# Tokens of the last chunk kept in their own order and stored by another queue; the first 1024 tokens gathered by index

## The reference

```python
# 1. attention: 16 neighbours on each side, and 24 blocks of 32 keys (max of k, mean of v)
x = attention(q, k, v)                       # 1536 tokens x 512
# 2. experts: each token goes to one of 8
expert_idx = np.argmax(logits, axis=1)
gate_w = probs[np.arange(N), expert_idx]
for e in range(E):
    mask = expert_idx == e
    h = np.maximum(x[mask] @ w1[e], 0.0)     # 512 -> 1024
    out[mask] = gate_w[mask, None] * (h @ w2[e])
# 3. one more network, the same for all tokens
h = x @ w_in                                 # 512 -> 2048
P = a[0] + a[1] * h + a[2] * h2 + a[3] * h3  # h2 = h*h, h3 = h2*h
Q = 1.0 + np.abs(b[0]) * np.abs(h) + np.abs(b[1]) * h2
return (P / (Q + 1e-06)) @ w_out             # 2048 -> 512
```

## Time and profile before

| | us |
|---|---|
| median of 3 runs | 735.77 |
| lowest and highest | 734.84 and 739.65 |
| the profiled execution | 735.92 |
| its span, from the first to the last instruction | 734.4 |
| mean granted clock of TensorE | 0.978 of 2.4 GHz |

### The profile page before, as it was taken

The page is one execution under the profiler, slowest core; times in us unless marked ns, Lnnn a source line. Parts: engine busy times, 40 slices in busy tenths (PEclk is TensorE's granted clock), DMA queues, the critical chain, the costliest instruction groups (busy, mean ns, idle before and its releaser), DMA issues.

```text
span 734.4 us, 11488 instructions
## 1 busy us (share of the span) xinstructions
PE 684.3 (93%) x3415; PEld 547.5 (75%) x3415; DVE 498.1 (68%) x976; ACT 417.7 (57%) x786; POOL 171.8 (23%) x232
## 2 busy tenths in 40 slices
PE   4779999999789999899999999999999999999991
PEld 4457777777567878688888888888888888888871
DVE  7566667676566787514314437999989899898881
ACT  5445565565346686424424546876667666666650
POOL 4358999431240103331020101000000010200002
PEclk9979999999899999999999999999999999999996
DMA  8374544311597699545622421101000010100001
GB/s 291 63 265 133 137 131 112 79 48 46 200 320 269 248 336 312 179 46 207 223 95 72 174 93 34 39 1 29 30 1 0 15 58 1 58 0 1 1 0 58
DMA packets 53780, 80.88 MB, mean 110 GB/s; under 512 B 31680, under 2 KB 31696, under 8 KB 52440
## 3 DMA queue, kind: packets, MB, share of 16 engines
q1 hardware_dynamic: 45288, 54.92, 23.3%
q0 software_dynamic: 7984, 25.20, 10.7%
q10 hardware_dynamic: 448, 0.02, 0.1%
HBM read 63.50 MB, written 16.63 MB: 109 GB/s over the span
## 4 chain that ended last, share of the span: by engine, by line
PE 81%; DMA 6%; DVE 5%; ACT 3%; issue 2%; SPq 1%; ACTq 1%; POOL 1%; DVEq 0%; POOLq 0%
PE bank L1612 18%; PE bank L1627 17%; PE bank L1580 11%; PE bank L1359 10%; PE bank L1559 10%; PE bank L1468 4%; PE bank L1442 4%; DMA raw_late<-in_moe_w_dram 3%; PE bank L1467 3%; DVE weights L1219 2%; DMA kraw<-in_k_dram 2%; ACT weights L798 2%; PE bank L1487 1%; PE bank L1375 1%; DMA x_by_slot<-x_all,slot_id 1%
## 5 line engine op out<-in xcount | busy, mean ns | idle before, releaser
L1627 PE MATMUL bank<-weights,G 128*128 128x512 f32 x576 | 140.6, 393 | 1.9 <-DVE G L1219 1.9
L1612 PE MATMUL bank<-X2T,weights 128*128 128x512 f32 x576 | 141.0, 394 | 0.0
L1627 PEld LDWEIGHTS bank<-weights,G 128*128 128x128 f32 x576 | 108.0, 188 | 27.2 <-DVE G L1219 2.6
L1612 PEld LDWEIGHTS bank<-X2T,weights 128*128 128x128 f32 x576 | 107.5, 188 | 23.7
L1580 PE MATMUL bank<-weights,HT 128*128 x456 | 111.1, 399 | 8.5 <-DVE HT L1219 8.5
L1559 PE MATMUL bank<-weights,XT 128*128 (+1 forms) x432 | 108.4, 399 | 2.4 <-DVE XT L1219 1.5
L1580 PEld LDWEIGHTS bank<-weights,HT 128*128 128x128 f32 x456 | 84.4, 188 | 28.5 <-issue 9.5
L1559 PEld LDWEIGHTS bank<-weights,XT 128*128 128x128 f32 x432 | 79.6, 188 | 21.0 <-DVE XT L1219 1.7
L850 ACT ACTIVATE qd<-bank,coef 128x512 f32<-128x512 f32 x48 | 33.1, 690 | 74.4 <-PE bank L1612 74.3
L1219 DVE TENSOR_TENSOR HT<-bank,HT 128x512 fp32r<-128x512 f32 x38 | 24.5, 686 | 70.1 <-ACT HT L878 68.3
L1219 DVE TENSOR_TENSOR weights<-raw_late,weights 128x2048 f32 (+1 forms) x20 | 41.3, 2076 | 23.6 <-ACT weights L798 23.6
(11 more groups left out here) (222 smaller groups left out, 1174.0 us busy)
## 6 DMA issues: line engine op xcount, KB each, us to landing
raw_early<-in_moe_w_dram SPq DMA_DIRECT2D x14, 1024.0 KB, 6.3
raw_late<-in_moe_w_dram SPq DMA_DIRECT2D x14, 1024.0 KB, 10.8
y_in_order<-yo POOLq DMA_DIRECT2D x19, 256.0 KB
x_all<-in_moe_w_dram POOLq DMA_DIRECT2D x8, 512.0 KB, 3.9
x_by_slot<-x_all SPq DMA_DIRECT2D x1, 3328.0 KB, 14.8
kraw<-in_k_dram SPq DMA_DIRECT2D x3, 1024.0 KB, 8.6
qraw<-in_q_dram SPq DMA_DIRECT2D x12, 256.0 KB, 4.3
x<-y_in_order POOLq DMA_DIRECT2D x12, 256.0 KB, 3.2
```

Of the source, the lines that this page charges most:

```text
L1612: last = T_.matmul(bank[6 + f % 2][:, :], W[:, 0, wa, kc * F2 + f * P:kc * F2 + (f + 1) * P], X2T[c % 2][:, xa, kc * C_TOK:(kc + 1) * C_TO ...
L1627: last = T_.matmul(bank[tt][:, :], G[:, f % 2, ga, tt * P:(tt + 1) * P], W[:, 1, wa, f * DM:(f + 1) * DM], start=(f == 0 and n_ == 0), sto ...
```

## The change

The chunks are cut in another way. The last chunk is now the last 512 tokens in the order of the tokens; the first two chunks are the first 1024 tokens, sorted by expert among themselves (`SORTED` = 8 tiles).

- All tiles are fetched from `y_in_order` by index, with an indirect DMA: the sorted ones by `y_row`, the last chunk's by `c_at`. The last chunk takes its gates straight from `gate_id`.
- `store_out` on POOL is left for the first two chunks. SP stores the last one with plain DMAs.
- `places` also works out `s_at`, the place among the sorted 1024 tokens, for which PE and DVE keep the count of the first 8 tiles (`early_count`). `gate_in_order` has three columns (gate, token, row in `y_in_order`) for 1024 tokens; its eight scatters go two behind each of tiles 4 to 7.
- The first chunk's rows may lie anywhere in the first 1024 rows, and wait for 15 stored tiles. Three are requested behind the store of tile 14; the fourth goes to `xg[0]`, once tile 18 has been transposed. Its request stands on POOL in front of the store of tile 16. The rows of tile 18 are requested before these. All four tiles are multiplied by their gates at the end of tile 16 and transposed in tile 17, into banks 6, 7, 4 and 0.

```diff
@@ constants and tiles
+        SORTED = NT - CT
+        gate_id = top.take("gate_id", [P, NT, 3], F32)
+        placed = top.take("placed", [P, SORTED, 3], F32)
...
-        FIRST_X2 = {MAXT - 4: (0, 1), MAXT - 3: (2,), MAXT - 2: (3,)}
@@ helpers
-        def x2_bank(c, tt):
-            return (6 if c == 0 else 4) + tt % 2
+        def x2_bank(T):
+            return (6, 7, 4, 0)[T] if T < CT else 4 + T % 2
+        def x2_tile(T):
+            if T < X2_SLOTS:
+                return x2[:, T, :]
+            return xg[0] if T == CT - 1 else x2[:, (T - CT) % X2_SLOTS, :]
@@ SP, at its end
+            for T in range(SORTED, NT):
+                sp.wait_ge((acc_dve, acc_act)[T % 2], T // 2 + 3)
+                sp.dma_start(out[T * P:(T + 1) * P, :], ost[:, T % CT, :]).then_inc(last_out, 16)
+            sp.wait_ge(last_out, 16 * CT)
@@ POOL
             def load_x2(T):
-                if T >= X2_SLOTS:
-                    pool.wait_ge(cx_mm, T - X2_SLOTS + 1)
-                pool.dma_start(x2[:, T % X2_SLOTS, :], ys[T * P:(T + 1) * P, :]).then_inc(x2_in[T % X2_SLOTS], 16)
+                if T == CT - 1:
+                    pool.wait_ge(bx_mm, MAXT)
+                elif T >= CT:
+                    pool.wait_ge(cx_mm, T - CT + 1 if T < CT + X2_SLOTS else T - X2_SLOTS + 1)
+                where = y_row[:, T:T + 1] if T < SORTED else c_at[:, T:T + 1]
+                G_.indirect_dma_start(out=x2_tile(T), out_offset=None, in_=ys[0:2 * C_TOK if T < CT else N, :],
+                                      in_offset=bass.IndirectOffsetOnAxis(ap=where, axis=0))\
+                  .then_inc(x2_extra if T == CT - 1 else x2_in[T if T < CT else (T - CT) % X2_SLOTS], 16)
...
-                if i + AHEAD < MAXT:
+                if i + AHEAD < MAXT - 1:
                     load_x(i + AHEAD)
                 store_y(i)
+                if i == MAXT - 5:
+                    load_x(MAXT - 1)
...
-                if FIRST_PLACED <= i < FIRST_PLACED + NT // 3:
-                    for T in range(3):
-                        place_gates(3 * (i - FIRST_PLACED) + T)
+                if FIRST_PLACED <= i < FIRST_PLACED + SORTED // 2:
+                    place_gates(2 * (i - FIRST_PLACED))
+                    place_gates(2 * (i - FIRST_PLACED) + 1)
...
-                if i == tiles_for(0) + 1:
+                if i == MAXT - 5:
+                    pool.wait_ge(token_ready, 1)
+                    pool.wait_ge(y_out, 16 * (MAXT - 4))
                     for T in range(X2_SLOTS):
                         load_x2(T)
                 if i == MAXT - 4:
-                    load_x2(X2_SLOTS)
-            for T in range(CT, NT):
-                pool.wait_ge(y_out, 16 * tiles_for(T // CT))
+                    load_x2(CT - 1)
+            pool.wait_ge(y_out, 16 * MAXT)
+            for T in range(CT, NT - 1):
                 load_x2(T)
-            pool.wait_ge(token_ready, 1)
-            for T in range(NT):
+            for T in range(CT):
+                store_out(T)
+            load_x2(NT - 1)
+            for T in range(CT, SORTED):
                 store_out(T)
@@ DVE, place
+                if T == SORTED:
+                    V.tensor_copy(early_count[:, :], bank[rank_bank(T)][:, (H + 1) * E:(H + 2) * E])
@@ DVE, places
-                V.tensor_copy(c_at[:, :], top1[:, :]).then_inc(c_at_ready, 1)
+                link(V.tensor_copy(c_at[:, :], top1[:, :]))
+                link(V.tensor_copy(gate_id[:, :, 2], top1[:, :]))
+                link(V.scalar_tensor_tensor(early_count[:, :], iota_e[:, 0, :], -float(REGION), early_count[:, :], ALU.mult, ALU.add))
+                pre = thr[:, :, 0:E]
+                link(V.tensor_tensor(pre, tri[:, :, :], early_count[:, :].unsqueeze(1).to_broadcast([P, E, E]), ALU.mult))
+                link(V.tensor_reduce(shift, pre, AX.X, ALU.add))
+                link(V.tensor_tensor(shift, shift, early_count[:, :], ALU.subtract))
+                link(V.tensor_tensor(shift, before, shift, ALU.subtract))
+                part = [P, SORTED, E]
+                link(V.tensor_tensor(LG2[:, 0:SORTED, :], oh[:, 0:SORTED, :], shift.unsqueeze(1).to_broadcast(part), ALU.mult))
+                link(V.tensor_reduce(first[:, 0:SORTED], LG2[:, 0:SORTED, :], AX.X, ALU.add))
+                link(V.tensor_tensor(first[:, 0:SORTED], top1[:, 0:SORTED], first[:, 0:SORTED], ALU.subtract))
+                V.tensor_copy(s_at[:, :], first[:, 0:SORTED]).then_inc(c_at_ready, 1)
@@ DVE, tile_b
-                for tt in FIRST_X2.get(i, ()):
-                    x2_lo(0, tt)
-                for tt in FIRST_X2.get(i + 1, ()):
-                    gated(tt)
+                if i == MAXT - 2:
+                    for tt in range(CT):
+                        x2_lo(0, tt)
...
+                if i == MAXT - 3:
+                    for T in range(CT):
+                        gated(T)
@@ PE, ranks
+                if T == SORTED:
+                    last = T_.matmul(b_[:, at + E:at + 2 * E], ones[:, :], seen[:, T % 2, :], start=True, stop=True)
@@ PE, x2_transposes and tile_b
-                if T == CT:
+                if T == 2:
                     pe.wait_ge(bx_lo, MAXT)
+                elif T == CT - 1:
+                    pe.wait_ge(relu_done, 2 * MAXT - 1)
...
-                for tt in FIRST_X2.get(i, ()):
-                    x2_transposes(0, tt)
+                if i == MAXT - 2:
+                    for tt in range(CT):
+                        x2_transposes(0, tt)
```

More of the change, by code:

```diff
@@ L102, in moe_mlp_kernel @@
         ident = top.take("ident", [P, P], F32)
-        gate_id = top.take("gate_id", [P, NT, 2], F32)
-        placed = top.take("placed", [P, NT, 2], F32)
-        token_of = top.take("token_of", [P, NT], U32)
+        SORTED = NT - CT
+        gate_id = top.take("gate_id", [P, NT, 3], F32)
+        placed = top.take("placed", [P, SORTED, 3], F32)
+        token_of = top.take("token_of", [P, SORTED], U32)
+        y_row = top.take("y_row", [P, SORTED], U32)
+        s_at = top.take("s_at", [P, SORTED], U32)
         slot_id = top.take("slot_id", [P, NT], U32)
@@ L163, in moe_mlp_kernel @@
         zidx = ra.take("zidx", [P, E], U32)
+        early_count = ra.take("early_count", [P, E], F32)
         upper = ra.take("upper", [P, P], BF16)
@@ L346, in rank_bank, with wait_x2 @@
             return 6 if T == NT - 2 else 7
-        def tiles_for(c):
-            return min(MAXT, (c + 1) * CT + E - 1)
-        def x2_bank(c, tt):
-            return (6 if c == 0 else 4) + tt % 2
+        def x2_bank(T):
[4 more added lines that the diff above has]
+            return xg[0] if T == CT - 1 else x2[:, (T - CT) % X2_SLOTS, :]
+        def wait_x2(eng, T):
+            if T == CT - 1:
+                eng.wait_ge(x2_extra, 16)
+            elif T < X2_SLOTS:
+                eng.wait_ge(x2_in[T], 16)
+            else:
+                eng.wait_ge(x2_in[(T - CT) % X2_SLOTS], 16 * ((T - CT) // X2_SLOTS + 2))
         def halves_of(f):
@@ L639, in place_gates @@
             def place_gates(T):
[L640 removed]
+                G_.indirect_dma_start(out=gs, out_offset=bass.IndirectOffsetOnAxis(ap=s_at[:, T:T + 1], axis=0),
                                       in_=gate_id[:, T, :], in_offset=None).then_inc(gates_out, 16)
             def load_x2(T):
[L644 to L646 removed]
+                if T == CT - 1:
+                    pool.wait_ge(bx_mm, MAXT)
[5 more added lines that the diff above has]
+                  .then_inc(x2_extra if T == CT - 1 else x2_in[T if T < CT else (T - CT) % X2_SLOTS], 16)
             def store_out(T):
@@ L826, in x2_hi @@
                 dst = X2T[c % 2][:, HI, :].rearrange("p (k n) -> p k n", k=KC)
-                A_.copy(dst[:, :, tt * P:(tt + 1) * P], bank[x2_bank(c, tt)][:, :].rearrange("p (k n) -> p k n", k=KC))\
+                A_.copy(dst[:, :, tt * P:(tt + 1) * P], bank[x2_bank(c * CT + tt)][:, :].rearrange("p (k n) -> p k n", k=KC))\
                   .then_inc(cx_hi, 1)
@@ L1230, in gated @@
             def gated(T):
-                r = T % X2_SLOTS
-                dve.wait_ge(placed_in, 16)
-                dve.wait_ge(x2_in[r], (T // X2_SLOTS + 1) * 16)
-                V.tensor_scalar(x2[:, r, :], x2[:, r, :], placed[:, T, 0:1], None, ALU.mult).then_inc(x2_gated, 1)
+                wait_x2(dve, T)
+                g_ = placed if T < SORTED else gate_id
+                V.tensor_scalar(x2_tile(T), x2_tile(T), g_[:, T, 0:1], None, ALU.mult).then_inc(x2_gated, 1)
             def x2_lo(c, tt):
```

23 lines of the change are left out of this document (14 added, 9 removed).

## The result

| | before | after |
|---|---|---|
| median | 736.21 us (6 runs, 732.67 to 739.65) | 728.96 us (6 runs, 726.94 to 730.15) |
| the profiled execution | 735.92 | 729.16 |
| its span | 734.4 | 727.7 |

The ratio is 0.9896, with a 95% interval of 0.9863 to 0.9930: about 7 us faster. The forecast was 735.7 us in a range of 732.0 to 739.0, with four small terms that cancel. In a later measurement, beside other kernels, it came out at 728.60 us, ratio 0.9900 (0.9874 to 0.9926).

A forecast was written before the change was run, and what follows sets the result against it. PE was taken as the bound almost everywhere. The terms -2.0 + 2.2 - 0.4 + 0.1 sum to -0.1 us, giving 735.8 us on the profiled execution and 735.7 us on the median, in a range of 732.0 to 739.0.

The forecast's parts named there:

- the first part: End of the kernel: last stores issued by SP instead of POOL, -2.0 us; the 8.4 us closing stretch left as is.
- Rival (c): End: SP's stores land no sooner than POOL's because the closing stretch waits for something else, 737.8 us; chance 0.09.
- The stores: Last chunk's stores from SP: 2.4 us taken, between 2.05 and 2.8, giving -2.0 us; they don't queue much.
- The index work: Behind tile 3: ten more DVE operations in `places` take 2.25 us, all added to PE's wait, +2.2 us.
- rival b: Before g2 of tile 4: PE's longer idle time halves the clock, 2.6 us lost, 738.4 us; chance 0.14.
- rival a: Tiles 4 to 7: the delay at tile 3 is absorbed by the queue of loads, 733.6 us; chance 0.20.
- The fewer scatters: Behind tiles 4 to 7: eight gate scatters instead of twelve, -0.4 us, between 0 and 1.3 saved.
- The attention stage: Attention stage: one more count of the first 1024 tokens on PE and DVE, +0.1 us, between 0 and 0.33.
- The first chunk's rows: Tiles 14 to 18: rows gathered by index and transposed in tile 17, 0 us, with 5.8 us of cover.
- The chunk stage: Second network: the other chunks' loads become gathers, 0 us; PE has 33 us between the last stored tile and their use.
- the forecast's own range: Whole kernel: the two main terms cancel, 734.3 to 737.3 us from the bounds on stores and scatters; chance 0.44.

The follow-up runs named there:

- e2: The changed kernel, with POOL waiting for SP's last stores as its last instruction and issuing nothing more: 736.95 us, ratio to the kernel before 1.0028.
- e1: The kernel before, with the last chunk's four stores issued by SP as plain DMAs into a DRAM tensor of their own: 725.23 us, ratio 0.9870.
- e3: The changed kernel, with the last of the four stores issued as a plain DMA by POOL, which waits for it: 737.76 us, ratio 1.0037.
- e9: The changed kernel with `places` behind tile 7, tiles aligned to 64 bytes and seven filler matmuls before PE's last group: 721.94 us, ratio 0.9828.

## Why the prediction was wrong

**The step that failed is the first part's sentence on the closing stretch**: "After that come 734.4 - 726.0 = 8.4 us in which no engine works; I leave them as they are." They belonged to POOL's end: its DRAIN from 726.6 to 734.2 stands in the trace of the kernel before, though not in its timeline. A wait alone brings them back (+8 us, e2), and moving POOL's last work away takes them out of a kernel that is otherwise the old one (-10 us, e1). From the last copy to the end it was -10.4 us instead of -2.0, and 7.6 of them are the closing stretch (8.4 to 0.8). Rival (c) saw that something else might hold the end, but only as a reason for less gain; none of the rivals was that the stretch could shrink, and so the range stopped 3 us short. What was left alone was the largest part of the end.

**The stores**: 2.1 us to landing, between the two bounds, where 2.4 was taken. Last copy to last data is 1.7 us, against 4.5 before: -2.8 measured, -2.0 forecast. The prediction put a time to the last data (POOL's 2.4) beside times to landing (2.05 and 2.8); by landings it is 2.7 for POOL's indirect stores and 2.1 for SP's. Some 0.7 of the -2.8 is owed to the half clock of this trace: with the last group at full clock (e2) it is 2.4 us and -2.1, and there the stores do queue, which the prediction thought they hardly would. So the -2.0 is met at full clock in part by luck, since the two errors nearly cancel. The Trainium skill (DMA: Bandwidth & Descriptors, Latency and other measured facts) gives about 0.6 us to the first byte of a DMA of SP and about 1 us to that of POOL, an estimated 0.4 us of difference. Plain stores of 256 KB fit that in e3, 2.4 us to landing from POOL and a median of 2.1 from SP; no row has the first byte itself.

**The index work**: the operations took 2.24 us (2.25 forecast) and lay on PE's path. That they stay whole was the wrong reason for about the right sum, and this is luck: the clock fell (rival b, 7.98 us for 24 matmuls), and tiles 6 and 7 took most of both back (rival a). +1.3 in the trace, +1.8 (0.1 to 3.6) by itself in timed runs, against +2.2. The clock fell in all seven traces in which PE waited 3.86 to 4.87 us there, and it fell as well behind a wait of 2.18 us in e1 and not behind one of 2.18 in e9; in the kernel before, a wait of 3.46 us had left it up. So the length of the wait alone doesn't decide, and that one row was no ground for the low chance of this rival. That it can fall behind a wait agrees with the Trainium skill (TensorE: Matmul & The Clock Gate, Part 1), by which an idle TensorE gets half the clock.

**The fewer scatters** (-0.4) were not measured by themselves. **The attention stage** (+0.1): the two traces differ by 0.1 us up to tile 3, but executions with the same code differ by up to 5 us there, so no run shows this term.

**The first chunk's rows**: 0 forecast, 0.05 us measured. From the gather's issue to the start of its gate it took 3.9 us, 3.6 forecast, and DVE was free 4.9 us before it was wanted again, 5.8 forecast.

**The chunk stage**: 0 forecast, +0.7 measured, by the place in SBUF and not by the gathers. No view of the kernel before could show this.

**The sums**: the forecast's own range comes out of its bounds as about 733.9 to 736.7 and not 734.3 to 737.3, and case (a) with the best stores as 732.7 and not 732. Neither moves the measured 728.96 into the range.

## What to carry to other kernels

Look at what lies behind the last data of the last store, and list the closing instructions of every engine: an idle-looking stretch of 8 us at the end was the biggest lever of this kernel, and one wait on POOL makes or removes it. Let POOL finish early; give the last stores to SP, and the last waits too. Small index work on DVE belongs where PE has no split or HT of it to wait for: `places` and its scatters cost 4 to 5 us more behind tile 3 than behind tile 7, where PE doesn't wait for them. When tables are added in front of big tiles, time again with the tiles moved back: the shift itself can cost or give as much as the edit.

## What the runs showed of the hardware that was not expected

- POOL closes with a DRAIN of 7.6 to 8.4 us in every trace, SP with one of at most 0.12. From POOL's last instruction to the end of the execution it is 8.0 us (issue without wait), and 8.4 to 8.7 us from the last data when it waits for that. SP: 0.7 to 0.8 us from the last data to the end.
- Matmuls of 128x512 in float32 halves at the same clock: 5.51 or 5.61 us for 24, 2.76 or 2.80 for 12 of `c1` and 2.77 or 2.74 for 12 of `c2`, by where the operands lie in SBUF (32 and 128 bytes apart).
- A wait of PE of 1.8 us in a dense stretch was followed by half clock in six of twelve traces.
